# Second product of a feed-forward block at full array height, the first product left at half height

## The chip, the cores and the metric

The kernel runs on one core of a Trainium2 chip. The metric is the device time of one execution, in microseconds (us). A span in the profile is the time from the first to the last instruction of the program on that core.

## The reference

What is computed is a per-position softmax over seven taps, a causal convolution of `x` with those taps, and then a feed-forward block whose gate is h times sigmoid(1.702 h):

```
w = softmax(weight_gen)                      # 4 x 4096 x 8 heads x 7 taps
conv[b,s,h,:] = sum_k w[b,s,h,k] * x_pad[b,s+k,h,:]     # 192 channels
h = conv.reshape(16384, 192) @ w_in          # 192 -> 2048
g = h * (1.0 / (1.0 + np.exp(-1.702 * h)))
out = g @ w_out                              # 2048 -> 192
```

The arithmetic must hold close to float32. The kernel splits every matrix operand into a high part rounded to `fp32r` and a low part, the remainder, and adds three products: high by high, high by low, low by high.

## The kernel before

**Pieces and units.** The 16,384 tokens are cut into 18 pieces (`PIECES`): four narrow ones, then fourteen wide ones. VectorE makes the convolution of the next piece while TensorE works on this one. A piece is processed in units: 8 in a narrow piece, 16 in a wide one, 256 in all. A unit takes 1024 columns, as two halves h of 512, through one hidden chunk of 128 for each half (in a wide piece every half meets its 16 chunks in 16 units).

**First product** (`first_product`, the matmul on L651). The 192 channels lie as three slices of 64 rows; the tokens of half 0 lie on partitions 0 to 63 and those of half 1 on partitions 64 to 127. So a matmul uses 64 rows of the array. Nine terms (three slices by three high and low combinations) by two halves are 18 matmuls of 64 rows by 512 columns for each unit. The matmuls of the two halves use different rows of the array and different banks of `hid`. I call two such neighbours a pair.

**Gate.** ScalarE reads `hid` twice (L316 writes `gate` in float32, L319 writes `gate_hi`), VectorE writes `gate_lo` (L565).

**Second product** (`second_product`). It contracts over the 128 partitions of `gate_hi` and `gate_lo`, and its 192 outputs with the split need two groups: `acc_main` (three terms) and `acc_rest` (two terms). The helper `halves` (L667) splits each of these contractions into rows 0 to 63 and rows 64 to 127. Five terms, by two halves h, by two halves of the rows, are 20 matmuls of 64 rows by 512 columns for each unit. In one pair the two row halves work on different h, so that they write different banks. First come the straight pairs (r equals h), then the crossed ones for each accumulator, and four semaphores (`main_straight`, `main_added`, `rest_crosswise`, `rest_added`) keep a pair from adding to a bank that the pair two groups earlier is still adding to.

**Order.** TensorE's program is written out at the end of its block: the first product of unit v, then the second product of unit v minus 2 (`LAG`). Only at the start and the end of a narrow piece, and at the end of all, do two units of the same product follow each other. TensorE waits for `gate_hi_ready` of two units earlier ahead of a first product and for `gate_lo_ready` of its own unit ahead of a second product.

**Other places the prediction speaks of.** At the start of the program four full-height float32 warm-up products run (L608), and twelve 128 by 128 transposes (L618), both with 128 rows. ScalarE copies their result (`xt`, L295) and VectorE does too (L515); the first products of L651 wait for these copies. At the end of a piece ScalarE (`lift`: L303, L307) and VectorE (L544, L549) read the accumulators out; ScalarE's part waits for `main_added` and then for `rest_added`.

Of the kernel before, what the change touches and what calls it, by code (L numbers as in the profile page):

```python
# [12 lines left out]
HALF = 64  # L13
# [24 lines left out]
def ffn_of_dynamic_conv(nc: bass.Bass, x_runs: bass.AP, tap_runs: bass.AP, x_first: bass.AP, tap_first: bass.AP,  # L38
# [34 lines left out]
    with ExitStack() as ctx:  # L73
        def sb(name, shape, dt=F32):
            return ctx.enter_context(nc.sbuf_tensor(name, shape, dt))

        def sem(name):
            return ctx.enter_context(nc.semaphore(name))
# [5 lines left out]
        w2 = sb("w2", [P, CH, 2 * D], F32R)  # L84
# [17 lines left out]
        gate_hi = sb("gate_hi", [P, SLOTS, 2, N], F32R)  # L102
        gate_lo = sb("gate_lo", [P, SLOTS, 2, N], F32R)
# [12 lines left out]
        acc_main = ctx.enter_context(nc.psum_tensor("acc_main", [P, 2, N], F32))  # L116
        acc_rest = ctx.enter_context(nc.psum_tensor("acc_rest", [P, 2, N], F32))
# [20 lines left out]
        xt_hi_ready, xt_lo_ready = sem("xt_hi_ready"), sem("xt_lo_ready")  # L138
        hid_ready = sem("hid_ready")
        gate_ready, gate_hi_ready, gate_lo_ready = sem("gate_ready"), sem("gate_hi_ready"), sem("gate_lo_ready")  # L140
        main_straight, rest_crosswise = sem("main_straight"), sem("rest_crosswise")
        main_added, rest_added = sem("main_added"), sem("rest_added")
        main_out_act, main_out_dve = sem("main_out_act"), sem("main_out_dve")
        rest_crossed, rest_out = sem("rest_crossed"), sem("rest_out")
# [5 lines left out]
        def wait(eng, s, value):  # L150
            if value > 0:
                eng.wait_ge(s, value)
# [3 lines left out]
        def is_narrow(j):  # L156
            return PIECES[j] == NARROW
# [4 lines left out]
        def closes_first(j):  # L162

            return 1 <= j <= 4
# [5 lines left out]
        def slice_of(h, k):  # L170

            return (k + h) % SLICES
# [3 lines left out]
        MAIN, MAIN_LO = slice(0, P), slice(2 * P, 3 * P)  # L176
        REST_COLS, REST_HI, REST_LO = slice(P, 2 * P), slice(P, D), slice(D, 2 * P)
# [422 lines left out]
        @block.tensor  # L600
        def _(pe):
            def turn_head():

                flat = x_head.rearrange("p t d -> p (t d)")
                pe.wait_ge(x_loaded, 16)
                pe.wait_ge(head_op, 5)
                for i in range(WARM_UP):
                    nc.tensor.matmul(hid[:, 0, 0, :], flat[:, i * P:(i + 1) * P], flat[:, N:2 * N], start=True, stop=True)  # L608
                pe.wait_ge(ident_loaded, 16)
                for k in range(SLICES):  # L610
                    if k < SLICES - 1:
                        pe.wait_ge(head_summed, k + 2)
                    else:
                        pe.wait_ge(head_again, 1)
                    for u in range(FIRST):

                        two = head_conv[:, u, k:k + 2, :].rearrange("p k c -> p (k c)")
                        last = nc.tensor.transpose(head_turned[k][:, u * P:(u + 1) * P], two, ident[:])  # L618
                    last.then_inc(head_turned_ready, 1)

            def first_product(j, v):
                n = UNIT0[j] + v
                q, cc = v // (CH // 2), v % (CH // 2)
                if n == UNIT0[len(NARROWS)] + CH // 2:
                    pe.wait_ge(w1_doubled, 64)
                wait(pe, gate_hi_ready, n - 1)
                f = slice(cc * P, (cc + 1) * P)
                terms = [(w, part, k) for w, part in ((w1_hi, 0), (w1_lo, 0), (w1_hi, 1)) for k in range(SLICES)]
                for i, (w, part, k) in enumerate(terms):
                    if n == 0:  # L630
                        if i == 1:
                            pe.wait_ge(head_hi_dve, 1)
                        elif i < SLICES:
                            pe.wait_ge(head_hi_act, 1 + i // 2)
                        elif i >= 2 * SLICES:
                            pe.wait_ge(head_lo, i - 2 * SLICES + 1)
                    if j > 0 and v == 0 and i == 0:
                        pe.wait_ge(xt_hi_ready, j)
                        if is_narrow(j):
                            pe.wait_ge(hi_crossed, 2 * j)  # L640
                    if j > 0 and v == 0 and i == 2 * SLICES:
                        pe.wait_ge(xt_lo_ready, j)
                        if is_narrow(j):
                            pe.wait_ge(lo_crossed, 2 * j)
                    if n in (0, 1, 2) and i == SLICES:
                        pe.wait_ge(w1_lo_ready, n + 1)
                    if n in (4, 6) and i == SLICES:
                        pe.wait_ge(w1_late_ready, n // 2 - 1)
                    for h in range(2):
                        rows = slice(h * HALF, (h + 1) * HALF)  # L650
                        last = nc.tensor.matmul(hid[:, v % 2, h, :], w[rows, k if j else slice_of(h, k), q, f],  # L651
                                                xt[rows, j % 2, part, k, :], start=(i == 0), stop=(i == len(terms) - 1))
                last.then_inc(hid_ready, 1)

            def second_product(j, v):
                n = UNIT0[j] + v
                s = v % SLOTS
                first, last_unit = v == 0, v == UNITS[j] - 1
                q, cc = v // (CH // 2), v % (CH // 2)
                chunk = (cc + q * (CH // 2), cc + (1 - q) * (CH // 2))  # L660

                def halves(acc, g, cols, crossed, start, stop):

                    for r in range(2):
                        h = 1 - r if crossed else r
                        rows = slice(r * HALF, (r + 1) * HALF)
                        done = nc.tensor.matmul(acc[:, h, :], w2[rows, chunk[h], cols], g[rows, s, h, :],  # L667
                                                start=start, stop=stop)
                    return done

                if n in (0, 2):
                    pe.wait_ge(w2_lo_ready, n + 2)
                if n == SOON:
                    pe.wait_ge(w2_late_ready, 2)
                wait(pe, gate_lo_ready, n + 1)
                if first:
                    wait(pe, main_out_act, j)
                    wait(pe, main_out_dve, j)

                wait(pe, main_added, n)  # L680
                halves(acc_main, gate_hi, MAIN, False, first, False)
                halves(acc_main, gate_hi, MAIN_LO, False, False, False)
                halves(acc_main, gate_lo, MAIN, False, False, False).then_inc(main_straight, 1)
                if first:
                    wait(pe, rest_out, 2 * j)
                wait(pe, rest_added, n)
                halves(acc_rest, gate_hi, REST_COLS, True, first, False)
                halves(acc_rest, gate_lo, REST_COLS, True, False, False).then_inc(rest_crosswise, 1)
                wait(pe, main_straight, n + 1)
                halves(acc_main, gate_hi, MAIN, True, False, False)  # L690
                halves(acc_main, gate_hi, MAIN_LO, True, False, False)
                halves(acc_main, gate_lo, MAIN, True, False, last_unit).then_inc(main_added, 1)
                wait(pe, rest_crosswise, n + 1)
                halves(acc_rest, gate_hi, REST_COLS, False, False, False)
                halves(acc_rest, gate_lo, REST_COLS, False, False, last_unit).then_inc(rest_added, 1)

            turn_head()
            for j in range(LAST + 1):
                if closes_first(j):
                    for v in range(UNITS[j - 1] - LAG, UNITS[j - 1] - (j in MIXED)):  # L700
                        second_product(j - 1, v)
                for v in range(UNITS[j]):
                    first_product(j, v)
                    if j in MIXED and v == 0:
                        second_product(j - 1, UNITS[j - 1] - 1)
                    elif v >= LAG:
                        second_product(j, v - LAG)
                    elif j > 0 and not closes_first(j):
                        second_product(j - 1, v - LAG + UNITS[j - 1])
            for v in range(UNITS[LAST] - LAG, UNITS[LAST]):  # L710
                second_product(LAST, v)
# [48 lines left out]
```

## Time and profile before

| | |
|---|---|
| median of 3 runs | 1128.13 us (1127.7 to 1128.32) |
| span of the profiled execution | 1125.8 us |
| TensorE matmuls | 9748, busy 1111.0 us (99% of the span) |
| TensorE weight loads | 9748, busy 916.4 us (81%) |
| VectorE, ScalarE | 802.1 us (71%), 621.4 us (55%) |

The profiled execution has no time of its own beside its span; the median of the runs is 2.3 us above that span. A matmul's busy time reaches from its start to its modelled end, and neighbours overlap, so the distance from one start to the next tells what a matmul costs, not its duration. PEld is the weight load, which overlaps PE. In the chain of work that ended last, 96% of the span lies on TensorE.

### The profile page before, as it was taken

What the parts mean: (1) busy time and instruction counts of PE and PEld (TensorE: products, weight loads), DVE (VectorE), ACT (ScalarE), POOL (GpSimd) and SP (SyncE); (2) the same over time, 40 slices, a digit from 0 to 9 for tenths busy, and PEclk for the clock granted to TensorE, in tenths of its full rate; (3) what the DMA queues carried; (4) which work ended last, traced back from release to release, by engine and by line L of the source; (5) the groups of instructions that cost most, each with busy time, mean ns of one, the idle gap of its engine ahead of it and who ended that gap; (6) DMA issues with size and microseconds to landing.
All of it is one profiled execution on the core that took longest, in us unless ns stands there. A gap on an engine that the chain in (4) does not pass through costs nothing.

```text
span 1125.8 us, 21691 instructions
## 1 busy us (share of the span) xinstructions
PE 1111.0 (99%) x9748; PEld 916.4 (81%) x9748; DVE 802.1 (71%) x710; ACT 621.4 (55%) x658; POOL 10.5 (1%) x11
## 2 busy tenths in 40 slices
PE   6999999999999999999999999999999999999998
PEld 4788888888888888888888888888888888888886
DVE  7899988587685866859668496785957768587322
ACT  7767655565545655455464555645555555454543
POOL 2000000000000000000000000000000000000000
PEclk9999999999999999999999999999999999999999
DMA  8801010101001010010100101010010100100000
GB/s 274 234 19 54 15 54 1 39 29 40 29 1 40 29 40 29 1 49 20 40 29 14 55 1 40 29 40 29 1 40 29 40 29 1 40 29 1 29 1 29
DMA packets 9948, 43.46 MB, mean 39 GB/s; under 512 B 1088, under 2 KB 2368, under 8 KB 7552
## 3 DMA queue, kind: packets, MB, share of 16 engines
q1 hardware_dynamic: 8400, 40.51, 10.7%
q0 software_dynamic: 1456, 1.57, 0.9%
q8 instruction: 77, 1.26, 0.5%
q14 instruction: 15, 0.12, 0.0%
HBM read 24.77 MB, written 12.58 MB: 33 GB/s over the span
## 4 chain that ended last, share of the span: by engine, by line
PE 96%; ACT 1%; DMA 1%; DVE 1%; issue 0%; POOL 0%; ACTq 0%; DVEq 0%; SPq 0%
PE hid L651 45%; PE acc_main L667 30%; PE acc_rest L667 20%; DMA taps<-w 1%; DMA gate<-in_x_first 0%; DVE hid L486 0%; DVE prod L480 0%; ACT gate_hi L319 0%; ACT gate L316 0%; ACT w L335 0%; ACT w L270 0%; ACT L316 0%; ACT L261 0%; PE acc_main L618 0%; DVE hid L480 0%
## 5 line engine op out<-in xcount | busy, mean ns | idle before, releaser
L316 ACT ACTIVATE gate<-hid 128x1024 f32<-128x1024 f32 x256 | 263.0, 1027 | 481.1 <-PE hid L651 480.5
L565 DVE TENSOR_TENSOR gate_lo<-gate,gate_hi 128x1024 fp32r<-128x1024 f32 x256 | 312.9, 1222 | 261.5 <-ACT gate_hi L319 261.5
L651 PE MATMUL hid<-xt,w_hi 64*128 64x512 f32 x3072 | 431.7, 387 | 0.0
L651 PEld LDWEIGHTS hid<-xt,w_hi 64*128 64x128 f32 x3072 | 288.2, 185 | 61.0 <-ACT gate_hi L319 0.8
L667 PE MATMUL acc_main<-gate_hi,w 64*128 64x512 f32 x2048 | 315.9, 387 | 0.8 <-ACT w L341 0.8
L319 ACT ACTIVATE gate_hi<-hid 128x1024 fp32r<-128x1024 f32 x256 | 261.1, 1020 | 0.0
L667 PEld LDWEIGHTS acc_main<-gate_hi,w 64*128 64x128 f32 x2048 | 192.1, 185 | 41.1 <-ACT w L341 1.2
L651 PE MATMUL hid<-xt,w_lo 64*128 64x512 f32 x1536 | 215.9, 387 | 0.0
L667 PE MATMUL acc_main<-gate_lo,w 64*128 64x512 f32 x1024 | 199.7, 387 | 0.0
L667 PE MATMUL acc_rest<-gate_hi,w 64*128 64x512 f32 x1024 | 199.6, 387 | 0.0
L667 PE MATMUL acc_rest<-gate_lo,w 64*128 64x512 f32 x1024 | 199.6, 387 | 0.0
L651 PEld LDWEIGHTS hid<-xt,w_lo 64*128 64x128 f32 x1536 | 144.3, 185 | 29.9
L410 DVE TENSOR_TENSOR conv<-conv,prod 128x1536 f32<-128x1536 f32 (+1 forms) x102 | 164.3, 1611 | 0.6
L403 DVE TENSOR_TENSOR prod<-xwin,tap_norm 128x1536 f32<-128x1536 f32 (+1 forms) x102 | 163.1, 1612 | 1.3 <-ACT xt L275 0.6
L667 PEld LDWEIGHTS acc_main<-gate_lo,w 64*128 64x128 f32 x1024 | 96.2, 184 | 20.0
L667 PEld LDWEIGHTS acc_rest<-gate_lo,w 64*128 64x128 f32 x1024 | 96.2, 184 | 20.0
L667 PEld LDWEIGHTS acc_rest<-gate_hi,w 64*128 64x128 f32 x1024 | 96.2, 185 | 19.9
L544 DVE COPY outs_main<-acc_main 128x512 f32<-128x512 f32 x14 | 9.7, 692 | 41.2 <-PE acc_main L667 41.2
L549 DVE TENSOR_TENSOR outs_rest<-acc_rest,outs_rest 64x512 f32<-64x512 f32 x36 | 23.0, 676 | 8.1 <-ACT outs_rest L307 8.1
L428 DVE STREAM_TRANSPOSE prod<-conv 128x1536 f32<-128x1536 f32 (+1 forms) x17 | 27.7, 1631 | 0.1
L436 DVE TENSOR_TENSOR xt<-prod,xt 128x1536 fp32r<-128x1536 f32 (+1 forms) x17 | 27.4, 1611 | 0.3 <-ACT xt L267 0.2
L403 DVE TENSOR_TENSOR conv<-xwin,tap_norm 128x1536 f32<-128x1536 f32 (+1 forms) x17 | 27.4, 1611 | 0.1
(57 smaller groups left out, 226.3 us busy)
## 6 DMA issues: line engine op xcount, KB each, us to landing
xwin<-in_x_runs SPq DMA_DIRECT2D x15, 1056.0 KB, 4.8
out<-outs_main SPq DMA_DIRECT2D x13, 512.0 KB, 2.6
out<-outs_rest SPq DMA_DIRECT2D x13, 256.0 KB, 2.9
taps<-in_tap_runs SPq DMA_DIRECT2D x1, 3136.0 KB, 14.6
taps<-in_w_rows SPq DMA_DIRECT2D x2, 1536.0 KB, 9.7
w_hi<-w_hi SPq DMA_DIRECT2D x2, 768.0 KB, 9.0
w_lo<-w_lo SPq DMA_DIRECT2D x2, 768.0 KB, 9.4
out<-outs_main SPq DMA_DIRECT2D x6, 256.0 KB, 2.1
```

The source lines that it names most:

```text
L316: nc.scalar.activation(gate[:, v % 2, :, :], hid[:, v % 2, :, :], ACT.Gelu_apprx_sigmoid).then_inc(gate_ready, 1)
L319: nc.scalar.activation(gate_hi[:, v % SLOTS, :, :], hid[:, v % 2, :, :], ACT.Gelu_apprx_sigmoid).then_inc(gate_hi_ready, 1)
L403: nc.vector.tensor_tensor(to.rearrange("p (g c) -> p g c", c=GRP), xwin[:, at:at + u, :].rearrange("p t (h c) -> p (t h) c", c=GRP), norm[ ...
L410: nc.vector.tensor_tensor(acc, acc, prod[:, k % 2, 0:u * CB], ALU.add).then_inc(conv_ready if last else conv_op, 1)
L428: nc.vector.transpose(turned(j).rearrange("p k (u i) -> p u k i", i=LANES), conv[:, 0:PIECES[j] * CB].rearrange("p (u k c) -> p u k c", k= ...
L436: nc.vector.tensor_tensor(own(j, 1), turned(j), own(j, 0), ALU.subtract).then_inc(xt_lo_ready, 1)
L544: nc.vector.tensor_copy(outs_main[:, 1, :], acc_main[:, 1, :]).then_inc(main_out_dve, 1)
L549: nc.vector.tensor_tensor(outs_rest[:, h, :], acc_rest[0:HALF, h, :], outs_rest[:, h, :], ALU.add).then_inc(rest_out, 1)
L565: nc.vector.tensor_tensor(gate_lo[:, v % SLOTS, :, :], gate[:, v % 2, :, :], gate_hi[:, v % SLOTS, :, :], ALU.subtract).then_inc(gate_lo_r ...
L651: last = nc.tensor.matmul(hid[:, v % 2, h, :], w[rows, k if j else slice_of(h, k), q, f], xt[rows, j % 2, part, k, :], start=(i == 0), sto ...
L667: done = nc.tensor.matmul(acc[:, h, :], w2[rows, chunk[h], cols], g[rows, s, h, :], start=start, stop=stop)
```

## The change

Every term of the second product is now one matmul over all 128 rows for each half h (`whole`), 10 for each unit instead of 20. All terms of `acc_main` come first, half 0 and then half 1, and then those of `acc_rest`. `main_added` is incremented after the sixth of the ten matmuls, `rest_added` after the tenth; the semaphores `main_straight` and `rest_crosswise` are gone, and so are the waits of TensorE on its own earlier work. The first product keeps its 18 matmuls of 64 rows.

```diff
-                def halves(acc, g, cols, crossed, start, stop):
-
-                    for r in range(2):
-                        h = 1 - r if crossed else r
-                        rows = slice(r * HALF, (r + 1) * HALF)
-                        done = nc.tensor.matmul(acc[:, h, :], w2[rows, chunk[h], cols], g[rows, s, h, :],
-                                                start=start, stop=stop)
-                    return done
+                def whole(acc, g, cols, h, start, stop):
+
+                    return nc.tensor.matmul(acc[:, h, :], w2[:, chunk[h], cols], g[:, s, h, :], start=start, stop=stop)
...
-                wait(pe, main_added, n)
-                halves(acc_main, gate_hi, MAIN, False, first, False)
-                halves(acc_main, gate_hi, MAIN_LO, False, False, False)
-                halves(acc_main, gate_lo, MAIN, False, False, False).then_inc(main_straight, 1)
+                for h in range(2):
+                    whole(acc_main, gate_hi, MAIN, h, first, False)
+                    whole(acc_main, gate_hi, MAIN_LO, h, False, False)
+                    done = whole(acc_main, gate_lo, MAIN, h, False, last_unit)
+                done.then_inc(main_added, 1)
                 if first:
                     wait(pe, rest_out, 2 * j)
-                wait(pe, rest_added, n)
-                halves(acc_rest, gate_hi, REST_COLS, True, first, False)
-                halves(acc_rest, gate_lo, REST_COLS, True, False, False).then_inc(rest_crosswise, 1)
-                wait(pe, main_straight, n + 1)
-                halves(acc_main, gate_hi, MAIN, True, False, False)
-                halves(acc_main, gate_hi, MAIN_LO, True, False, False)
-                halves(acc_main, gate_lo, MAIN, True, False, last_unit).then_inc(main_added, 1)
-                wait(pe, rest_crosswise, n + 1)
-                halves(acc_rest, gate_hi, REST_COLS, False, False, False)
-                halves(acc_rest, gate_lo, REST_COLS, False, False, last_unit).then_inc(rest_added, 1)
+                for h in range(2):
+                    whole(acc_rest, gate_hi, REST_COLS, h, first, False)
+                    done = whole(acc_rest, gate_lo, REST_COLS, h, False, last_unit)
+                done.then_inc(rest_added, 1)
```

TensorE's program where the first unit's second product stands between two first products, before (shapes are those of the output, `w` stands for `w2`; L651 is the first product, L667 the second):

```order
L651 MATMUL hid<-xt,w_hi 128x512 x6
L667 MATMUL acc_main<-gate_hi,w 128x512 x4
L667 MATMUL acc_main<-gate_lo,w 128x512 x2
L667 MATMUL acc_rest<-gate_hi,w 128x512 x2
L667 MATMUL acc_rest<-gate_lo,w 128x512 x2
L667 MATMUL acc_main<-gate_hi,w 128x512 x4
L667 MATMUL acc_main<-gate_lo,w 128x512 x2
L667 MATMUL acc_rest<-gate_hi,w 128x512 x2
L667 MATMUL acc_rest<-gate_lo,w 128x512 x2
L651 MATMUL hid<-xt,w_hi 128x512 x6
```

The same place of the changed kernel (L650 is the first product, L663 the second):

```order
L650 MATMUL hid<-xt,w_hi 128x512 x6
L663 MATMUL acc_main<-gate_hi,w 128x512 x2
L663 MATMUL acc_main<-gate_lo,w 128x512
L663 MATMUL acc_main<-gate_hi,w 128x512 x2
L663 MATMUL acc_main<-gate_lo,w 128x512
L663 MATMUL acc_rest<-gate_hi,w 128x512
L663 MATMUL acc_rest<-gate_lo,w 128x512
L663 MATMUL acc_rest<-gate_hi,w 128x512
L663 MATMUL acc_rest<-gate_lo,w 128x512
L650 MATMUL hid<-xt,w_hi 128x512 x6
```

The 20 matmuls of 64 rows have become 10 of 128 rows, and a matmul of 64 rows still stands on either side. Over the whole program the row height now changes 249 times from a first to a second product and 248 times back, counted in the order that the program writes; before, it is 64 rows from the first L651 to the end.

The end of TensorE's program, the last unit, with its semaphore waits, before:

```order
L667 MATMUL acc_main<-gate_hi,w 128x512 [waits main_added,gate_lo_ready]
L667 MATMUL acc_main<-gate_hi,w 128x512 x3
L667 MATMUL acc_main<-gate_lo,w 128x512 x2
L667 MATMUL acc_rest<-gate_hi,w 128x512 [waits rest_added]
L667 MATMUL acc_rest<-gate_hi,w 128x512
L667 MATMUL acc_rest<-gate_lo,w 128x512 x2
L667 MATMUL acc_main<-gate_hi,w 128x512 [waits main_straight]
L667 MATMUL acc_main<-gate_hi,w 128x512 x3
L667 MATMUL acc_main<-gate_lo,w 128x512 x2
L667 MATMUL acc_rest<-gate_hi,w 128x512 [waits rest_crosswise]
L667 MATMUL acc_rest<-gate_hi,w 128x512
L667 MATMUL acc_rest<-gate_lo,w 128x512 x2
```

And in the changed kernel:

```order
L663 MATMUL acc_main<-gate_hi,w 128x512 [waits gate_lo_ready]
L663 MATMUL acc_main<-gate_hi,w 128x512
L663 MATMUL acc_main<-gate_lo,w 128x512
L663 MATMUL acc_main<-gate_hi,w 128x512 x2
L663 MATMUL acc_main<-gate_lo,w 128x512
L663 MATMUL acc_rest<-gate_hi,w 128x512
L663 MATMUL acc_rest<-gate_lo,w 128x512
L663 MATMUL acc_rest<-gate_hi,w 128x512
L663 MATMUL acc_rest<-gate_lo,w 128x512
```

The four waits on TensorE's own work are gone, and the last matmul of `acc_main` now stands four matmuls ahead of the end instead of two pairs.

## Rows read from the trace of the kernel before

**Rows 1.** The page: span and busy time; granted clock in 40 slices.

```profile
span 1125.8 us, 21691 instructions
...
PE 1111.0 (99%) x9748; PEld 916.4 (81%) x9748; DVE 802.1 (71%) x710; ACT 621.4 (55%) x658; POOL 10.5 (1%) x11
...
PEclk9999999999999999999999999999999999999999
```

**Rows 2.** The page: the chain that ended last, by engine and by line.

```profile
PE 96%; ACT 1%; DMA 1%; DVE 1%; issue 0%; POOL 0%; ACTq 0%; DVEq 0%; SPq 0%
PE hid L651 45%; PE acc_main L667 30%; PE acc_rest L667 20%; DMA taps<-w 1%; DMA gate<-in_x_first 0%; DVE hid L486 0%; DVE prod L480 0%; ACT gate_hi L319 0%; ACT gate L316 0%; ACT w L335 0%; ACT w L270 0%; ACT L316 0%; ACT L261 0%; PE acc_main L618 0%; DVE hid L480 0%
```

**Rows 3.** Waits: engine line waited for, us in total, times, longest.

```profile
ACT gate L316 <- PE hid L651: 480.5, 230, 4.7
DVE gate_lo L565 <- ACT gate_hi L319: 261.5, 168, 3.5
...
PE hid L608 <- DVE hid L480: 7.1, 1, 7.1
...
PE acc_main L618 <- DVE outs_main L508: 2.0, 1, 2.0
...
PE acc_main L667 <- ACT w L341: 0.8, 1, 0.8
```

**Rows 4.** Windows of 500 us: each engine's busy time and instructions, clock.

```profile
core 0: us, PE busy (x) PEld busy (x) DVE busy (x) ACT busy (x) POOL busy (x), PEclk, DMA share, GB/s
100.00:600.00 500.00, 500.00 (x4414) 414.26 (x4412) 374.48 (x314) 279.54 (x295) 0.00 (x0) 1.00 0.09 30
```

**Rows 5.** Timeline, 500.0 to 500.4 us: start, length, engine.

```profile
499.85 0.39 PE L667 MATMUL acc_rest<-gate_hi,w 64*128 64x512 f32 x2
499.85 0.19 PEld L667 LDWEIGHTS acc_rest<-gate_lo,w 64*128 64x128 f32 x2
500.07 0.39 PE L667 MATMUL acc_rest<-gate_lo,w 64*128 64x512 f32 x2
...
500.30 0.39 PE L651 MATMUL hid<-xt,w_hi 64*128 64x512 f32 x2
```

**Rows 6.** Timeline, 10.5 to 11.95 us: weight loads of the warm-up.

```profile
10.55 0.19 PEld L608 LDWEIGHTS hid<-gate 128*128 128x128 f32 x1 [0.38 <-issue]
10.98 0.19 PEld L608 LDWEIGHTS hid<-gate 128*128 128x128 f32 x1 [0.24 <-issue]
11.41 0.19 PEld L608 LDWEIGHTS hid<-gate 128*128 128x128 f32 x1 [0.24 <-issue]
```

**Rows 7.** Timeline of PE and PEld, 14.3 to 15.9 us: last transposes, first pair.

```profile
15.29 0.60 PE L618 MATMUL acc_rest<-ident,outs_main 128*128 128x128 f32 x4
...
15.51 0.14 PEld L618 LDWEIGHTS acc_rest<-ident,outs_main 128*128 128x128 f32 x1
...
15.62 0.27 PE L618 MATMUL acc_rest<-ident,outs_main 128*128 128x128 f32 x1
...
15.82 0.18 PEld L651 LDWEIGHTS hid<-xt,w_hi 64*128 64x128 f32 x2 [0.17 <-ACT xt L295]
15.82 0.50 PE L651 MATMUL hid<-xt,w_hi 64*128 64x512 f32 x2
```

**Rows 8.** Timeline: releasers of exposed loads, and those loads.

```profile
15.06 0.60 ACT L295 ACTIVATE xt<-acc_main 128x512 fp32r<-128x512 f32 x1 [0.69 <-PE acc_main L618]
15.50 0.69 DVE L515 CAST xt<-acc_main 128x512 fp32r<-128x512 f32 x1 [0.45 <-PE acc_main L618]
...
16.24 0.19 PEld L651 LDWEIGHTS hid<-xt,w_hi 64*128 64x128 f32 x2 [0.23 <-DVE xt L515]
...
19.50 1.02 ACT L319 ACTIVATE gate_hi<-hid 128x1024 fp32r<-128x1024 f32 x1
...
20.57 0.50 PE L651 MATMUL hid<-xt,w_hi 64*128 64x512 f32 x2
20.57 0.19 PEld L651 LDWEIGHTS hid<-xt,w_hi 64*128 64x128 f32 x2 [0.40 <-ACT gate_hi L319]
```

**Rows 9.** Windows of 1 us around TensorE's early idle time.

```profile
13.00:14.00 1.00, 0.00 (x0) 0.00 (x0) 0.97 (x3) 1.00 (x2) 0.00 (x0) 1.00 1.11 442
14.00:15.00 1.00, 0.61 (x6) 0.64 (x7) 1.00 (x3) 0.37 (x2) 0.69 (x1) 1.00 1.00 403
```

**Rows 10.** Timeline, 1118 to 1126 us: the last accumulators are read.

```profile
1120.48 0.60 ACT L303 ACTIVATE outs_main<-acc_main 128x512 f32<-128x512 f32 x1 [4.45 <-PE acc_main L667]
...
1120.50 0.39 PE L667 MATMUL acc_rest<-gate_lo,w 64*128 64x512 f32 x2
1121.10 1.08 ACT L307 ACTIVATE outs_rest<-acc_rest 64x512 f32<-64x512 f32 x2
```

More of the change, by code:

```diff
@@ L140, in ffn_of_dynamic_conv @@
         gate_ready, gate_hi_ready, gate_lo_ready = sem("gate_ready"), sem("gate_hi_ready"), sem("gate_lo_ready")
-        main_straight, rest_crosswise = sem("main_straight"), sem("rest_crosswise")
         main_added, rest_added = sem("main_added"), sem("rest_added")
```

## The prediction

> **What bounds the kernel now.** I read the page first: TensorE is busy in 99% of the span of 1125.8 us, VectorE in 71% and ScalarE in 55% [rows 1]. Busy shares can mislead, so the chain that ended last comes next: 96% of it is TensorE, of which 45% is the first product and 50% the second [rows 2]. The waits say the same from the other side: ScalarE waited 480.5 us for `hid` from TensorE and VectorE 261.5 us for ScalarE, while the longest sums of TensorE's own waits are 7.1 and 2.0 us at the start and 0.8 us for the late part of `w2` [rows 3]. So whatever one matmul costs from its start to the next one's start comes straight out of, or goes straight into, the span, and the other engines have room for either.
>
> That cost is read from a window: 4414 matmuls in 500 us, the clock granted in full (the level of 2.4 GHz) [rows 4]. That is 2207 pairs, 0.2266 us each. The timeline shows the same steps: pairs start at 499.85, 500.07 and 500.30 [rows 5]. 512 columns at 2.4 GHz are 0.2133 us, so a pair has 0.0133 us on top of its stream of columns. The next pair's weight loads start with the pair that is running and take 0.19 us [rows 5]: they are hidden, and this also holds at the border from the second product to the first, where both are 64 rows high. Check of the sum: a unit has 9 + 10 = 19 pairs, 4.305 us, and 256 units are 1102 us; the start and the end make the rest of the span.
>
> The sums below are made against the span of 1125.8 us; the median of the runs is 2.3 us above it, and I carry that over unchanged.
>
> **The change, part one: pairs become whole matmuls.** 2560 pairs of 64 rows become 2560 matmuls of 128 rows (256 units by 10). No row shows a full-height `fp32r` matmul of 512 columns. From below its step is bound by the stream, 0.2133 us; from above by the pair's 0.2266 us, if what a pair has on top is not due to its being two. Two kinds of rows lie near. The last three steps of the full-height transposes are (15.62 - 15.29) / 3 = 0.11 us each, with a load of 0.14 us that overlaps its neighbour [rows 7]: full-height loads do run under a full-height matmul, and faster than needed here, which excludes a loss from them. The loads of the float32 warm-up come every 0.43 us [rows 6], and twice 0.2133 is 0.427, so that what is on top is about 0.003 us for each instruction. I take 0.216 us. The saving is 2560 x (0.2266 - 0.216) = 27.1 us, with bounds 0 and 34 us.
>
> **Part two: the row height now alternates.** The order has 249 changes from 64 to 128 rows and 248 back, 497 in all; before, there was none after the start. A border of heights is shown only once in the trace, at the start: the last transpose (128 rows) starts at 15.62 and its columns are through one step later, at 15.73; the first pair of 64 rows starts its load at 15.82 [rows 7]. What held it? The profile names ScalarE's `xt`, which ended at 15.06 + 0.60 = 15.66 [rows 8]. But two controls show how soon a load starts after such a release where the height doesn't change: VectorE's cast ended at 16.19, the load started at 16.24; ScalarE's `gate_hi` ended at 20.52, the load started at 20.57 [rows 8]. Both are 0.05 us, so `xt` would have let the load go at 15.71. It came at 15.82, which is 0.09 us after the transposes' columns were through. I read the 0.09 us as emptying the array before its row height changes. Then the load was exposed: the first pair took 0.50 us in the record where a pair with a hidden load takes 0.39 us [rows 5, 7], and the control at 20.57, with no change of height, also has 0.50 us [rows 8]. So an exposed load costs 0.11 us.
>
> The price of one change of height by these rows is 0.09 + 0.11 us from the end of the columns to the next stream; from it goes what a step has on top anyway, about 0.01 us. That is 0.19 us, and 497 x 0.19 = 94.4 us. The bounds are wide, since it is one border, with a semaphore wait in the same place and from transposes rather than products. From below it is 0: the wait explains all of the delay, and the next load is prefetched as now. From above, emptying lasts to the record's end of a matmul, 0.387 - 0.213 = 0.174 us after its columns, and the load follows: 0.174 + 0.11 - 0.01 = 0.27 us, or 136 us in all. I take the value in between because it is the only one measured at a border. The change pays only below 27.1 / 497 = 0.055 us for each border.
>
> On a rule: the Trainium skill ("TensorEngine Tiling (Array Packing)", "Key Properties") says that a change of tiling mode, as against a change of tile, drains TensorE. It gives no price; by it the 0.09 us is no accident of the wait. For the load, "TensorE: Matmul & The Clock Gate" ("LDWEIGHTS (loading the stationary operand)") gives the columns divided by 1.2, which is 107 ns for 128 columns; the exposed 0.11 us agrees. Its section "Back-to-back issue gap" gives 215.7 ns for a full-height step of 512 columns in the warm state, by which part one would save 27.9 us; no run so far shows that step.
>
> **Part three: what costs nothing.** The removed waits of TensorE on itself (four in each unit) were met when reached: in the steady state no idle time stands ahead of L667 beyond the 0.8 us for `w2` [rows 3]. ScalarE and VectorE get a longer unit, not a shorter one, and wait for TensorE already [rows 3]; cover is needed only if the unit becomes shorter, and their 279.54 and 374.48 us of 500 [rows 4] leave room for the 2.5% by which it could. Gaps of 0.2 us can't be expected to lower the granted clock, since it stayed at 1.00 through more than 1 us without a matmul [rows 9]. At the very end `main_added` comes earlier relative to the last matmul: now L303 starts at 1120.48 and holds ScalarE until 1121.08, while the last pair of `acc_rest` ends at 1120.89 [rows 10]. Afterwards four matmuls, 0.86 us, stand behind the last of `acc_main`, L303 is done sooner, and L307 starts about 0.15 us earlier. This is the one further gain.
>
> **The sum.** 1125.8 - 27.1 + 94.4 - 0.15 = 1193.0 us of span, and 1195.3 us of time. I forecast 1195 us, about 6% slower. A unit in the steady state goes from 4.305 to 9 x 0.2266 + 10 x 0.216 + 2 x 0.19 = 4.58 us.
>
> **The rivals.**
>
> *The borders are free (faster).* The load for the other height is prefetched like any other, and the array need not be empty. Then only part one is left: 1128.1 - 27.1 - 0.15 = 1101 us. For it: a load that starts with the matmul before it is the rule in every row of the steady state, and the delay at 15.82 had a wait in it. Against it: the two controls of 0.05 us. It decides below 0.055 us for each border. Chance 0.12.
>
> *Only one of the two pieces is paid.* Either the load goes ahead in the shadow and the array is only emptied, or nothing is emptied and the load alone is exposed: about 0.10 us for each border, 50 us, and 1128.1 - 27.1 + 50 = 1151 us. For it: at 15.82 the instruction before the load was held by a semaphore, so that the trace can't say whether a load that is ready could have gone earlier. Chance 0.20.
>
> *The whole pipeline is emptied.* 0.27 us for each border: 1128.1 - 27.1 + 136 = 1237 us. For it: a stream of products of 512 columns may need longer to end than one transpose; against it, at 15.82 the record of the transpose still ran, to 15.62 + 0.27 = 15.89 [rows 7], when the load of the pair started. Chance 0.18.
>
> *The pair's extra 0.0133 us stays with whole matmuls, or the two directions of a border differ.* This moves the sum by up to 27 us either way and doesn't change its sign; it belongs to the range.
>
> **How the numbers follow.** My forecast's case (0.15 to 0.23 us for each border, 1175 to 1215 us) has 0.43, the full emptying 0.18, the half price 0.20, free borders 0.12; the remaining 0.07 is for prices between them or above. The range of 1140 to 1245 us takes in all but the free borders and what is beyond the upper bound. Differences within 0.2% (2.3 us), about what a measurement of this kernel can tell from no change, need a price of 0.05 to 0.06 us: 0.03. Faster 0.12, slower 0.85.
>
> **What the changed kernel's profile would show.** Part one: inside a second product, starts 0.216 us apart, one matmul each, with the load still under the one before; 0.2266 us would refute it. Part two: at a border the load starts about 0.30 us after the last matmul's start (0.2133 + 0.09), not together with it, and the first matmul behind it is recorded at about 0.50 us; starts across the border lie 0.41 us apart. If loads still start with the matmul before, the free case or the half price is right. Busy time of weight loads would fall, since ten of a unit's 38 are gone and these overlapped. Part three: ScalarE's and VectorE's waits for TensorE grow by about the added time, TensorE's own do not, and the granted clock stays at 1.00. The prediction is wrong if the border costs under 0.08 or over 0.29 us, and wholly so under 0.055 us.

## The result: 10.4% slower, and the profile after

The changed kernel takes 1245.86 us (median of 3 runs, 1245.49 to 1245.9) against 1128.13 us: a ratio of 1.1044, with a 95% interval of 1.1029 to 1.1059. The loss of 117.7 us has the forecast sign and lies 0.9 us beyond the top of the forecast range.

From the page of the changed kernel, the lines that answer to [rows 1, 2]:

```profile
span 1243.7 us, 16301 instructions
PE 1230.3 (99%) x7188; PEld 877.1 (71%) x7188; DVE 806.3 (65%) x710; ACT 621.3 (50%) x658; POOL 10.5 (1%) x11
...
PEclk9999999999999999999999999999999999999999
...
PE 98%; DVE 1%; DMA 0%; DVEq 0%; ACT 0%; issue 0%; SPq 0%
PE hid L650 47%; PE acc_main L663 33%; PE acc_rest L663 19%; DMA gate<-in_x_first 0%; DVE hid L485 0%; DVE prod L479 0%; PE acc_main L617 0%; DVE hid L479 0%; DVE outs_main L507 0%; DVE outs_rest L548 0%; ACT outs_rest L306 0%; DVEq L73 0%; PE acc_rest L617 0%; SPq L197 0%; DVEq L488 0%
```

TensorE executes 7188 matmuls instead of 9748, is as busy as before by share, and still bounds the kernel. Busy time doesn't tell of the loss, since it includes what a matmul waits for inside its record. The waits do, beside [rows 3]:

```profile
ACT gate L315 <- PE hid L650: 600.2, 232, 5.1
DVE gate_lo L564 <- ACT gate_hi L318: 366.9, 199, 3.9
PEld acc_main L663 <- issue: 86.4, 245, 0.4
...
PEld hid L650 <- issue: 85.3, 232, 0.4
```

ScalarE's wait for `hid` grew from 480.5 to 600.2 us, 119.7 us more, about the whole loss of 117.7 us, seen from an engine that has time. The two rows of weight loads are new. "issue" means that the profile shows nothing that held them. There are 245 and 232 of them; 4 more gaps ahead of `acc_main` are put down to VectorE's `gate_lo` and 18 ahead of `hid` to ScalarE's `gate_hi`, 2 of which stood at the start before as well. That makes 249 and 248, the changes of row height, and none had such a gap in the steady state before.

TensorE's timeline over one unit of the changed kernel, to be set beside [rows 5] (start, length, engine, merged where neighbours are alike):

```profile
504.26 0.73 PE L663 MATMUL acc_main<-gate_hi,w 128*128 128x512 f32 x2
504.83 0.40 PE L663 MATMUL acc_main<-gate_lo,w 128*128 128x512 f32 x1
...
506.45 0.40 PE L663 MATMUL acc_rest<-gate_lo,w 128*128 128x512 f32 x1
506.78 0.97 PE L650 MATMUL hid<-xt,w_hi 64*128 64x512 f32 x6
507.59 0.85 PE L650 MATMUL hid<-xt,w_lo 64*128 64x512 f32 x6
508.28 0.84 PE L650 MATMUL hid<-xt,w_hi 64*128 64x512 f32 x6
509.05 0.50 PE L663 MATMUL acc_main<-gate_hi,w 128*128 128x512 f32 x1
```

A unit lasts from 504.26 to 509.05, 4.79 us; 19 steps of 0.2266 us were 4.305 us. The 0.485 us on top is shared by two borders (changes of row height): 0.24 us each. The whole loss divided by all borders says the same: 117.7 / 497 = 0.237 us. The weight loads show the border from the other side, here ahead of the first product of the unit before:

```profile
501.99 0.30 PEld L650 LDWEIGHTS hid<-xt,w_hi 64*128 64x128 f32 x4 [0.37 <-issue]
```

The last whole matmul had started at 501.67. A load that is prefetched (sent ahead while the matmul before its own still runs) starts with that matmul; this one starts 0.32 us later, which is 0.11 us after the 0.2133 us of columns have passed.

The granted clock stays at 1.00:

```profile
600.00:1100.00 500.00, 500.00 (x2924) 356.35 (x2922) 317.50 (x261) 243.26 (x256) 0.00 (x0) 1.00 0.08 27
```

2924 matmuls at 28 for each unit are 104.4 units, 4.788 us each.

### The profile page after: what moved, and what is told of

Its sections match the earlier page's. It is cut to its first block, busy times and chain, and to the rows that moved or that the text cites. A ratio compares the mean times of both kernels' runs of the same rounds, so it can differ in the third digit from the quotient of the medians.

```text
span 1243.7 us, 16301 instructions
## 1 busy us (share of the span) xinstructions
PE 1230.3 (99%) x7188; PEld 877.1 (71%) x7188; DVE 806.3 (65%) x710; ACT 621.3 (50%) x658; POOL 10.5 (1%) x11
## 4 chain that ended last, share of the span: by engine, by line
PE 98%; DVE 1%; DMA 0%; DVEq 0%; ACT 0%; issue 0%; SPq 0%
PE hid L650 47%; PE acc_main L663 33%; PE acc_rest L663 19%; DMA gate<-in_x_first 0%; DVE hid L485 0%; DVE prod L479 0%; PE acc_main L617 0%; DVE hid L479 0%; DVE outs_main L507 0%; DVE outs_rest L548 0%; ACT outs_rest L306 0%; DVEq L73 0%; PE acc_rest L617 0%; SPq L197 0%; DVEq L488 0%
## 5 line engine op out<-in xcount | busy, mean ns | idle before, releaser
L315 ACT ACTIVATE gate<-hid 128x1024 f32<-128x1024 f32 x256 | 263.0, 1027 | 600.8 <-PE hid L650 600.2
L650 PE MATMUL hid<-xt,w_hi 64*128 64x512 f32 x3072 | 462.0, 406 | 0.0
L650 PEld LDWEIGHTS hid<-xt,w_hi 64*128 64x128 f32 x3072 | 268.7, 184 | 137.4 <-issue 85.3
L663 PE MATMUL acc_main<-gate_hi,w 128*128 128x512 f32 x1024 | 345.7, 418 | 0.0
L663 PEld LDWEIGHTS acc_main<-gate_hi,w 128*128 128x128 f32 x1024 | 172.7, 188 | 112.5 <-issue 86.4
L650 PE MATMUL hid<-xt,w_lo 64*128 64x512 f32 x1536 | 218.6, 389 | 0.0
L663 PE MATMUL acc_rest<-gate_hi,w 128*128 128x512 f32 x512 | 202.7, 396 | 0.0
L663 PE MATMUL acc_main<-gate_lo,w 128*128 128x512 f32 x512 | 202.2, 395 | 0.0
L663 PE MATMUL acc_rest<-gate_lo,w 128*128 128x512 f32 x512 | 201.2, 393 | 0.0
L650 PEld LDWEIGHTS hid<-xt,w_lo 64*128 64x128 f32 x1536 | 144.1, 184 | 33.6
L663 PEld LDWEIGHTS acc_main<-gate_lo,w 128*128 128x128 f32 x512 | 95.9, 187 | 22.7
L663 PEld LDWEIGHTS acc_rest<-gate_hi,w 128*128 128x128 f32 x512 | 96.1, 188 | 21.9
L663 PEld LDWEIGHTS acc_rest<-gate_lo,w 128*128 128x128 f32 x512 | 96.2, 188 | 21.2
```

Source lines behind the costliest of these rows:

```text
L315: nc.scalar.activation(gate[:, v % 2, :, :], hid[:, v % 2, :, :], ACT.Gelu_apprx_sigmoid).then_inc(gate_ready, 1)
L663: return nc.tensor.matmul(acc[:, h, :], w2[:, chunk[h], cols], g[:, s, h, :], start=start, stop=stop)
```

## The experiments

All ratios and differences are against runs of the kernel before on the same chip (medians 1127.83 us for the first four kernels, 1128.01 for the next four, 1127.91 for the last two). At this point my account was: a border costs about 0.20 us above a normal step, and a whole matmul steps in about 0.232 us.

**1. Fewer borders: two units at a time (`by_two`).**

```diff
+                if j > 4:
+                    for v in range(0, UNITS[j], 2):
+                        first_product(j, v)
+                        first_product(j, v + 1)
+                        for u in (v - LAG, v - LAG + 1):
+                            second_product(j if u >= 0 else j - 1, u if u >= 0 else u + UNITS[j - 1])
+                    continue
```

> The changed kernel with two first products, then two second products in each of the 13 last wide pieces; same matmuls, 208 fewer changes of row height. Theory 1 (a change of height costs about 0.20 us above a normal step, read from the changed kernel's steps): 208 x 0.20 = 42 us less, about 1203 us. Theory 2 (the loss is in the whole matmuls themselves, wherever they stand): 1246 us unchanged. Theory 3 (longer runs of whole matmuls also step faster, 0.216 instead of 0.232 us): about 1203 minus up to 33, so 1170 to 1190 us.

Measured: 1196.88 us, ratio 1.0613 (1.0597 to 1.0629). That is 49.0 us less than the changed kernel with the same matmuls: 208 borders fewer, 0.236 us each. Theory 2 is refuted. Theory 1 undervalued the border.

**2. and 3. The same matmuls with two borders and with four (`two_borders`, `four_borders`).** In both, `acc_rest` is made of pairs again and `acc_main` of whole matmuls. The second product with four borders:

```diff
+                halves(acc_rest, gate_hi, REST_COLS, True, first, False)
+                whole(acc_main, gate_hi, MAIN, 0, first, False)
+                whole(acc_main, gate_hi, MAIN_LO, 0, False, False)
+                whole(acc_main, gate_lo, MAIN, 0, False, last_unit)
+                halves(acc_rest, gate_lo, REST_COLS, True, False, False).then_inc(rest_crosswise, 1)
+                whole(acc_main, gate_hi, MAIN, 1, first, False)
...
+                halves(acc_rest, gate_hi, REST_COLS, False, False, False)
+                halves(acc_rest, gate_lo, REST_COLS, False, False, last_unit).then_inc(rest_added, 1)
```

With two borders both crossed pairs stand ahead of the six whole matmuls.

> Of each second product the four matmuls of acc_rest are four pairs of 64 rows again, two ahead of the whole matmuls of acc_main and two behind them; still two changes of height in a unit. Theory 1 (each border 0.20 us, a whole step 0.232 and a pair step 0.2266 us): 4 x 256 x 0.0054 = 5.5 us less than the changed kernel, about 1240 us. If borders alone count, 1246 us.

> The same matmuls as in the kernel with two borders (six whole, four pairs of the second product), but ordered so that the height changes four times in a unit. Theory 1: two more borders in each of 256 units, 512 x 0.20 = 102 us more than the kernel with two borders, about 1342 us. Rival (the loss lies in the whole matmuls, or in the change between the two products rather than in the height): no more than 1245 us.

Measured: 1251.47 us (ratio 1.1097, 1.1078 to 1.1115) and 1365.62 us (1.2109, 1.2091 to 1.2127). The difference is 114.2 us for 512 borders, 0.223 us each, though every matmul is the same. The border is the cost, and it costs about the same between the two products and inside one. Shown for the kernel with four (L667 pairs, L673 whole):

```profile
500.67 0.42 PE L667 MATMUL acc_rest<-gate_hi,w 64*128 64x512 f32 x2
501.02 0.73 PE L673 MATMUL acc_main<-gate_hi,w 128*128 128x512 f32 x2
501.59 0.40 PE L673 MATMUL acc_main<-gate_lo,w 128*128 128x512 f32 x1
501.92 0.49 PE L667 MATMUL acc_rest<-gate_lo,w 64*128 64x512 f32 x2
502.34 0.74 PE L673 MATMUL acc_main<-gate_hi,w 128*128 128x512 f32 x2
```

The single pair between two borders occupies TensorE from 501.92 to 502.34, 0.42 us instead of 0.227. The kernel with two borders missed its expectation of 1240 us: it is 5.6 us slower than the changed kernel. Not its steady unit is to blame, which is shorter, 4.760 us instead of 4.787:

```profile
700.16 0.73 PE L673 MATMUL acc_main<-gate_hi,w 128*128 128x512 f32 x2
...
704.92 0.73 PE L673 MATMUL acc_main<-gate_hi,w 128*128 128x512 f32 x2
```

The average over 500 us (3338 matmuls at 32 for each unit, 4.793 us) hides this, since it holds idle time of TensorE, 1.08 us by its busy time:

```profile
600.00:1100.00 500.00, 498.92 (x3338) 355.31 (x3339) 318.12 (x260) 243.62 (x256) 0.00 (x0) 1.00 0.08 27
```

The trace has twenty stalls that the changed kernel lacks, each with over 0.54 us from one start to the next, such as this one:

```profile
560.99 0.21 PEld L667 LDWEIGHTS acc_rest<-gate_hi,w 64*128 64x128 f32 x2 [0.55 <-issue]
```

Thirteen stand at the start of a piece, where `acc_rest` now comes first and must have been read out. Seven stand where two second products adjoin, and the wait for `rest_added` meets a pair that was only just issued. The profile names no releaser for most of them, so that the cause is read from their places. Each lengthens its unit by about 0.43 us (5.2 us from 709.68 to 714.88, instead of 4.76), some 8.7 us in all. Besides, each second product now has two borders of its own, also where two of them adjoin: 512 borders instead of 497, at 0.223 us some 3.3 us. The steady units give back 256 x 0.027 = 6.9 us. My estimate from these is 5.1 us more than the changed kernel, near the 5.6 measured. The expectation had none of the three.

**4. Alternating banks (`banks`).**

```diff
-                for h in range(2):
-                    whole(acc_main, gate_hi, MAIN, h, first, False)
-                    whole(acc_main, gate_hi, MAIN_LO, h, False, False)
-                    done = whole(acc_main, gate_lo, MAIN, h, False, last_unit)
+                for h in range(2):
+                    whole(acc_main, gate_hi, MAIN, h, first, False)
+                for h in range(2):
+                    whole(acc_main, gate_hi, MAIN_LO, h, False, False)
+                for h in range(2):
+                    done = whole(acc_main, gate_lo, MAIN, h, False, last_unit)
```

> The changed kernel with its whole matmuls alternating between the banks of half 0 and half 1, where it has three or two in a row into one bank. If adding to one bank in a row makes the whole step 0.232 instead of 0.216 us: up to 2560 x 0.016 = 41 us less, 1205 us. If the bank doesn't matter: 1246 us.

Measured: 1245.83 us against 1245.86. The order of the banks plays no part.

**5. No border at all, everything at full height (`all_whole`).**

```diff
-                    for h in range(2):
-                        rows = slice(h * HALF, (h + 1) * HALF)
-                        last = nc.tensor.matmul(hid[:, v % 2, h, :], w[rows, k if j else slice_of(h, k), q, f],
-                                                xt[rows, j % 2, part, k, :], start=(i == 0), stop=(i == len(terms) - 1))
+                    last = nc.tensor.matmul(hid[:, v % 2, i % 2, :], w[:, k, q, f], xt[:, j % 2, part, k, :],
+                                            start=(i < 2), stop=(i >= len(terms) - 2))
```

> The changed kernel with its first product at full height as well: nine matmuls of 128 rows for each unit in place of nine pairs, alternating between the two halves of hid, so that the first product sums other rows than the reference's. There is no change of height left, and each unit has 19 steps as before the change. Theory 1 (in a long run a whole matmul steps in 0.2267 us as a pair does, and the borders are the entire loss): 1128 us, as the kernel before. Theory 2 (a whole step is 0.232 us everywhere): 19 x 256 x 0.0054 = 26 us more, 1154 us. Theory 3 (0.216 us, as I had predicted): 52 us less, 1076 us.

Measured: 1127.55 us, ratio 0.9997 (0.9987 to 1.0006), the same as before. The timeline shows even steps over both products:

```profile
499.74 0.39 PE L661 MATMUL acc_main<-gate_lo,w 128*128 128x512 f32 x1
499.96 0.39 PE L661 MATMUL acc_rest<-gate_hi,w 128*128 128x512 f32 x1
500.19 0.39 PE L661 MATMUL acc_rest<-gate_lo,w 128*128 128x512 f32 x1
500.42 0.39 PE L661 MATMUL acc_rest<-gate_hi,w 128*128 128x512 f32 x1
500.64 0.39 PE L661 MATMUL acc_rest<-gate_lo,w 128*128 128x512 f32 x1
500.87 0.84 PE L648 MATMUL hid<-xt,w_hi 128*128 128x512 f32 x3
...
600.00:1100.00 500.00, 500.00 (x2208) 414.01 (x2207) 332.80 (x270) 261.69 (x275) 0.00 (x0) 1.00 0.08 25
```

2208 matmuls in 500 us are 0.2264 us each (one matmul more or less would change that by 0.0001 us), where a pair had 0.2266. A whole matmul costs what a pair costs, to within 0.1%. Both theories of another step, my prediction's 0.216 us and the 0.232 us that I had read from the changed kernel, fall here.

**6. Runs of 20 whole matmuls (`twice`).**

```diff
-                for h in range(2):
+                for t, h in ((0, 0), (0, 1), (1, 0), (1, 1)):
-                    whole(acc_main, gate_hi, MAIN, h, first, False)
+                    whole(acc_main, gate_hi, MAIN, h, first and t == 0, False)
```

(and alike for the other terms).

> The changed kernel with every term of the second product added twice, so that its output is twice the reference's: runs of 20 whole matmuls instead of 10, the same 497 borders. Theory 1 (steps settle at 0.2267 us about nine matmuls behind a border): 2560 x 0.2267 = 580 us more than the changed kernel, about 1826 us, and steps 10 to 18 of a run at 0.2267 us. Theory 2 (0.232 us everywhere): 1840 us. Theory 3 (0.216 us once settled): 1799 us.

Measured: 1824.18 us. One run of the second product in the timeline:

```profile
500.27 0.73 PE L663 MATMUL acc_main<-gate_hi,w 128*128 128x512 f32 x2
500.84 0.40 PE L663 MATMUL acc_main<-gate_lo,w 128*128 128x512 f32 x1
...
502.45 0.62 PE L663 MATMUL acc_main<-gate_hi,w 128*128 128x512 f32 x2
...
504.71 0.39 PE L663 MATMUL acc_rest<-gate_lo,w 128*128 128x512 f32 x1
505.03 0.97 PE L650 MATMUL hid<-xt,w_hi 64*128 64x512 f32 x6
```

From the tenth matmul (502.45) to the twentieth (504.71) there are ten steps in 2.26 us, 0.226 us each. In the changed kernel, whose run ends with the tenth, the seven steps from 504.83 to 506.45 take 0.231 us each. So steps are slow only for a while behind a border, and that while belongs to the border's price. How long it is differs: in the pairs of the changed kernel's first product the steps have settled after six, in its run of ten whole matmuls not by the last. This is why I had read 0.232 us as the step of a whole matmul.

**7. and 8. Shorter streams (`short_whole`, `short_pairs`).** The line in `whole`, and the same limit in `halves`:

```diff
+                    n_cols = N if first else 384
-                    return nc.tensor.matmul(acc[:, h, :], w2[:, chunk[h], cols], g[:, s, h, :], start=start, stop=stop)
+                    return nc.tensor.matmul(acc[:, h, 0:n_cols], w2[:, chunk[h], cols], g[:, s, h, 0:n_cols], start=start, stop=stop)
```

> The changed kernel with 384 instead of 512 columns in the matmuls of the second product, except in the first unit of a piece, so the last quarter of the columns lacks terms; 238 units, 2380 matmuls. If a step is the stream of its columns plus a constant of 0.013 us: 2380 x 0.0533 = 127 us less than the changed kernel, about 1119 us. If a step is bound by the weight load or by the issue of instructions: 1246 us unchanged.

> The same cut to 384 columns in the kernel before, with pairs of 64 rows; the last quarter of the columns lacks terms. If a pair's step is the stream of its columns plus 0.013 us: 2380 x 0.0533 = 127 us less than before, about 1001 us. If the pair's 0.2266 us is set by its four instructions (two loads, two matmuls) or by the load: 1128 us unchanged.

Measured: 1115.22 us for whole matmuls, 130.6 us less than the changed kernel, and 1030.06 us for pairs, 98 us less than before. The whole matmuls follow the columns closely, the pairs in the main. Whole matmuls of 384 columns in the timeline:

```profile
700.19 0.33 PE L664 MATMUL acc_rest<-gate_hi,w 128*128 128x384 f32 x1
700.36 0.34 PE L664 MATMUL acc_rest<-gate_lo,w 128*128 128x384 f32 x1
700.54 0.33 PE L664 MATMUL acc_rest<-gate_hi,w 128*128 128x384 f32 x1
700.71 0.34 PE L664 MATMUL acc_rest<-gate_lo,w 128*128 128x384 f32 x1
```

Three steps in 0.52 us are 0.173 us each, 0.160 of it stream: the same 0.013 us on top as with 512 columns. The pairs settle at the same 0.173 us. Neither the load (0.19 us, longer than this step) nor the number of instructions (two for a whole matmul, four for a pair) sets the step. The pairs gained 29 us less than expected. Their first product, whose matmuls still have 512 columns and no border near, runs in the slower steps:

```profile
702.05 0.86 PE L651 MATMUL hid<-xt,w_hi 64*128 64x512 f32 x6
702.75 0.85 PE L651 MATMUL hid<-xt,w_lo 64*128 64x512 f32 x6
703.44 0.85 PE L651 MATMUL hid<-xt,w_hi 64*128 64x512 f32 x6
```

Six steps in 1.39 us are 0.232 us each. Summed over the trace, slow steps of this kind cost about 14 us. About as much again is lost in stalls and in what follows on them: TensorE is nearer to its suppliers (5.9 us of waits for `gate_lo`, 4.8 us for the reading of `acc_rest`), and behind two waits for `gate_lo`, of 2.2 and 2.1 us, the granted clock falls:

```profile
84.00:87.00 3.00, 3.00 (x20) 2.35 (x18) 2.96 (x4) 0.12 (x1) 0.00 (x0) 0.60 0.00 0
```

Steps of 512 columns then take up to 0.427 us, twice 0.2133 us, which is the lower level, 1.2 GHz. The slow steps matter for the next experiment: here they come with no change of height and no exposed load before them, only behind shorter matmuls.

**9. A load exposed without a change of height (`self_wait`).** The kernel before, with:

```diff
                 last.then_inc(hid_ready, 1)
+                if j > 0:
+                    pe.wait_ge(hid_ready, n + 1)
```

> The kernel before, all 64 rows, with one wait added: behind each first product (248 units, all but the first piece) TensorE waits for that product's own completion. The next load can then not be prefetched although the height stays. Theory (a load that isn't prefetched costs 0.11 us and leaves the next few steps at 0.231 instead of 0.2267 us whatever held it back): record of a matmul 0.387 + release 0.05 + load 0.11 - a step 0.227 + 0.02 afterwards = 0.34 us, 248 x 0.34 = 84 us more, 1212 us, with steps of 0.224 to 0.236 us behind the wait. Rival (the slow steps belong to the change of height): steps of 0.2267 us behind the wait, 1207 us.

Measured: 1220.13 us, ratio 1.0817 (1.0799 to 1.0835): 92.2 us for 248 waits, 0.372 us each. All products are of 64 rows, and the load behind the wait starts 0.45 us after the last pair of the first product did:

```profile
503.21 0.84 PE L651 MATMUL hid<-xt,w_hi 64*128 64x512 f32 x6
504.12 0.30 PEld L669 LDWEIGHTS acc_main<-gate_hi,w 64*128 64x128 f32 x4 [0.48 <-PE hid L651]
504.12 0.72 PE L669 MATMUL acc_main<-gate_hi,w 64*128 64x512 f32 x4
504.68 0.40 PE L669 MATMUL acc_main<-gate_lo,w 64*128 64x512 f32 x2
...
506.53 0.84 PE L651 MATMUL hid<-xt,w_hi 64*128 64x512 f32 x6
```

From 504.68 to 506.53 are eight steps in 1.85 us, 0.231 us each. The slow steps follow here too, so they don't need a change of height. A load that came late is enough; by experiment 8 it isn't the only thing that brings them about. The expectation of 84 us had them too small (0.02 us); at eight steps and more they are 0.04 us, and the rest of the shortfall comes from the stall itself (0.451 us from start to start, where 0.387 + 0.05 was expected).

**10. Borders the other way round (`whole_first`).** The edit of experiment 5 made in the kernel before: the first product whole, the second in pairs.

> The kernel before with only its first product at full height: nine matmuls of 128 rows in place of nine pairs, summing other rows than the reference's; the second product keeps its ten pairs. 497 changes of height, in the opposite sense. Theory 1 (a border costs 0.236 us with its consequences, and whole matmuls and pairs step alike): 1245 us, as the changed kernel. Rival (what costs is the second product at full height): 1128 us.

Measured: 1245.51 us, ratio 1.1041 (1.1025 to 1.1058): within 0.4 us of the changed kernel, also with 497 borders. It is not the second product at full height that costs, but that the two heights differ.

## Why the prediction was right in its mechanism and wrong in its size

**What bounds the kernel** was right: TensorE's steps go straight into the span, and ScalarE's wait grew by 119.7 us while the time grew by 117.7.

**Part two, the border, was the right mechanism.** The forecast signs are all in the changed kernel's trace: the load starts 0.32 us after the last matmul's start (0.30 forecast), the first matmul behind it is recorded at 0.50 us, and the gaps number what the order has as changes (249 and 248). The comparison of experiments 2 and 3 shows the border as the cause with the matmuls held fixed, experiment 5 takes the borders away and the whole loss with them, experiment 10 turns them round and gets the same time. Free borders, and the half price, are refuted: both pieces are paid at every border. The full emptying that the prediction priced isn't seen either: the new load starts 0.32 us after the last matmul's start, before the record of that matmul has ended (0.40 us, a modelled end), and also before a load that waits for the last product to report itself done, 0.45 us in experiment 9. That the wait at the border is for an emptying of the array is an interpretation; the runs show only that it ends 0.11 us after the last columns, with 384 columns (0.27 us from start to start) as with 512.

**Its price was too small: 0.19 us against 0.237.** The two pieces that I had summed are nearly right (0.11 us from the end of the columns to the load instead of 0.09, and 0.11 us for the load). What was left out is what comes after: five to nine steps of about 0.231 us instead of 0.2266, some 0.03 us for each border. That term was not in the sum at all, although the trace of before shows it: behind the load at 20.57 us, the control of [rows 8], and one exposed step, the five steps from 20.91 to 22.07 us take 0.231 us each. 497 x 0.047 = 23 us.

**Part one was the larger error: a saving of 27.1 us that doesn't exist.** The step that failed is "I take 0.216 us". I had carried the overhead of 0.003 us of float32 warm-up products over to `fp32r` products, and treated the pair's 0.013 us as the price of being two. Experiment 5 measures the step of a whole matmul at 0.2264 us, the pair's, so neither my 0.216 us nor the 215.7 ns that stands beside it in the prediction is met. My bound of no saving was the true value, and I had chosen near the other end. There was a nearer row than those of the warm-up: the pair itself, of the same type and column count.

**The sum.** 1195.3 + 27.1 + 23 = 1245.4 us, against 1245.86 measured. This agreement is no separate proof, since the 0.237 us is the whole loss divided by the borders; the price that experiment 1 gives by itself, 0.236 us, leads to the same sum within 1 us. The forecast was low because both errors went the same way. The dearest case that the prediction priced, 1237 us, still had the full saving taken off, and the range ended at 1245; both bad bounds together give 1126 + 136 + 2 = 1264 us. That the measured time lies within 1 us of that end is chance.

**Part three** held. No waits of TensorE for other engines were added beyond those that fall on borders, and the clock stayed at 1.00. The end of the program gained what was forecast: the last reading of `acc_rest` by ScalarE starts 0.43 us after the last matmul's start (1238.99 against 1238.56), where it was 0.60 us before [rows 10].

Left open: why steps are slow for five to nine matmuls behind a late load or behind shorter matmuls, why the next load isn't prefetched across a border, and what the 0.013 us above the stream is. Of the kernels with whole matmuls that sum what the reference sums, the fastest is `by_two` at 1196.88 us. Even the one without any border, `all_whole`, only equals the kernel before, so I expect no gain over pairs from another grouping.

## What to carry to other kernels

Two facts go together when half-height pairs and full-height matmuls of `fp32r` are weighed: a pair over both halves of the rows costs as much as one full-height matmul, so full height saves nothing where pairs are already dense; and each change between the heights costs about a whole step (0.24 us here, where a step takes 0.2266), so where one product must be of half height, cut its neighbour to the same height or group the work so that the height changes seldom. When a term rests on a row of another data type, keep the bound of "no difference" as the value until a row of the same type says otherwise, and build the range from all bad bounds at once.

## What the runs showed of the hardware

- A step of `fp32r` products is the stream of columns plus 0.013 us, for 64 rows in pairs and for 128 rows alike, and at 384 columns as at 512 (0.173 and 0.2266 us, once settled).
- A change between 64 and 128 rows, in either direction, costs 0.223 to 0.237 us (experiments 1 to 3, and the whole loss over 497): the load starts about 0.11 us after the last columns, is exposed for 0.11 us, and the next steps are slow.
- Behind a load that wasn't prefetched, also without a change of height (experiment 9), steps average 0.231 us for five to nine matmuls and then settle at 0.2266 us (experiment 6). They are as slow behind shorter matmuls whose loads were prefetched (experiment 8, 0.232 us).
- A wait of TensorE for its own last matmul costs 0.372 us (experiment 9), more than a border.
